# Decay and phase sums: matrix products replaced by scans with features on partitions, in a fused attention and MLP kernel

## The reference

```python
for t in range(S):
    new_re = ar * S_re - ai * S_im
    new_im = ar * S_im + ai * S_re
    kv = np.einsum('bhd,bhe->bhde', k[:, :, t], v[:, :, t])
    S_re, S_im = (new_re + kv, new_im)
    y[:, :, t] = np.einsum('bhd,bhde->bhe', q[:, :, t], S_re)
```

## Time and profile before

| what | value |
|---|---|
| three runs | 1012.15, 1011.91 and 1009.15 us, median 1011.91 |
| the profiled execution | 1009.13 us, its span 1007.3 us |
| mean granted TensorE clock | 0.989 |
| TensorE, matmul busy | 960.0 us, 95% of the span |
| VectorE, ScalarE, GpSimd busy | 528.4, 422.3 and 364.9 us |
| moved by DMA | 66.84 MB |

### The profile page before, as it was taken

The page is one execution under the profiler, slowest core; times in us unless marked ns, Lnnn a source line. Parts: engine busy times, 40 slices in busy tenths (PEclk is TensorE's granted clock), DMA queues, the critical chain, the costliest instruction groups (busy, mean ns, idle before and its releaser), DMA issues.

```text
span 1007.3 us, 15116 instructions
## 1 busy us (share of the span) xinstructions
PE 960.0 (95%) x5913; PEld 877.4 (87%) x5913; DVE 528.4 (52%) x669; ACT 422.3 (42%) x674; POOL 364.9 (36%) x296
## 2 busy tenths in 40 slices
PE   6887699999999999999999999999999999999997
PEld 3556699999999999999999999999888888888886
DVE  5669869669669669669669654242212121212110
ACT  4364554554555554554554533363222121212121
POOL 0353543543543552543553533253222222222221
PEclk9999799999999999999999999999999999999999
DMA  9254411311311221221221020421001010101000
GB/s 352 69 167 117 149 40 41 104 46 40 98 53 40 84 68 40 79 71 41 71 80 40 24 79 25 160 99 42 15 1 63 1 63 1 63 1 63 1 32 33
DMA packets 55913, 66.84 MB, mean 66 GB/s; under 512 B 4896, under 2 KB 50208, under 8 KB 55840
## 3 DMA queue, kind: packets, MB, share of 16 engines
q1 hardware_dynamic: 55840, 65.84, 20.5%
HBM read 45.37 MB, written 11.01 MB: 56 GB/s over the span
## 4 chain that ended last, share of the span: by engine, by line
PE 80%; issue 7%; DVE 5%; ACT 3%; POOL 3%; DMA 1%; SPq 1%; ACTq 0%; POOLq 0%; DVEq 0%
PE acc L737 15%; PE hb L717 14%; PE hb L916 10%; PE acc L938 8%; PE bR L916 5%; PE bQ L916 5%; PE bR L830 3%; POOL gL L1310 3%; PE bP L938 2%; PE bR L801 2%; PE acc L864 2%; PE bQ L801 2%; PE bQ L823 2%; PE bQ L820 2%; PE bQ L784 1%
## 5 line engine op out<-in xcount | busy, mean ns | idle before, releaser
L1310 POOL TENSOR_TENSOR gL<-g_sb,gH 128x384 fp32r<-128x384 f32 x128 | 155.4, 1214 | 253.5 <-ACT gH L1016 209.5
L717 PE MATMUL hb<-xHL,winH 128*128 128x384 f32 x768 | 162.8, 347 | 3.9 <-DMA xHL<-yHL 3.9
L1358 POOL TENSOR_TENSOR pL<-p_sb,pH 128x512 fp32r<-128x512 f32 x48 | 67.0, 1395 | 232.0 <-ACT pH L1098 232.0
L717 PEld LDWEIGHTS hb<-xHL,winH 128*128 128x128 f32 x768 | 133.6, 191 | 5.0 <-DMA xHL<-yHL 4.6
L1230 DVE SCALAR_TENSOR_TENSOR g_sb<-t_sb,hb 128x384 f32<-128x384 f32 x128 | 70.2, 549 | 123.7 <-ACT t_sb L1034 72.1
L737 PE MATMUL acc<-gH,woutH 128*128 128x384 f32 x384 | 129.1, 336 | 4.1 <-ACT gH L1016 2.6
L737 PE MATMUL acc<-gH,woutL 128*128 128x384 f32 x384 | 128.6, 335 | 0.0
L737 PE MATMUL acc<-gL,woutH 128*128 128x384 f32 x384 | 128.3, 334 | 0.0
L1034 ACT ACTIVATE t_sb<-hb,cst 128x384 f32<-128x384 f32 x128 | 74.5, 582 | 89.7 <-PE hb L717 89.5
L1016 ACT CAST gH<-g_sb 128x384 fp32r<-128x384 f32 x128 | 65.4, 511 | 86.5 <-DVE g_sb L1230 85.7
L717 PE MATMUL hb<-xHL,winL 128*128 128x384 f32 x384 | 87.7, 336 | 0.0
(11 more groups left out here) (163 smaller groups left out, 2000.2 us busy)
## 6 DMA issues: line engine op xcount, KB each, us to landing
xHL<-yHL SPq DMA_DIRECT2D x48, 144.0 KB, 2.6
AR<-in_a_re_dram SPq DMA_DIRECT2D x8, 576.0 KB, 3.9
AI<-in_a_im_dram SPq DMA_DIRECT2D x8, 576.0 KB, 5.1
q_sb<-in_q_dram SPq DMA_DIRECT2D x24, 192.0 KB, 2.5
...
```

The lines of the kernel that those rows point to most:

```text
L717: mm = pe.matmul(o, w[:, kk * DF1 + ft * P:kk * DF1 + (ft + 1) * P], xv(u)[:, 2 * kk + part, :], start=(i == 0), stop=(i == 8))
L1310: pool.tensor_tensor(gL[:, (n % 3) * UNIT:(n % 3 + 1) * UNIT], g_sb[:, :], gH[:, (n % 3) * UNIT:(n % 3 + 1) * UNIT].bitcast(F32), ALU.subt ...
L1358: pool.tensor_tensor(pL[:, (n % 3) * UNIT2:(n % 3 + 1) * UNIT2], p_sb[:, (n % 2) * UNIT2:(n % 2 + 1) * UNIT2], pH[:, (n % 3) * UNIT2:(n % ...
```

## The change

The preparation is laid out with **features on partitions** and tokens along the columns (inputs `a_re_x`, `a_im_x`, `qk_x` are laid out so outside the kernel). A sum over tokens is then a scan along the columns on VectorE: three of 384 columns for the decays and three for the angles of a unit, in `pre` steps 6 and 10. `decay_sums`, `halves_sums`, `angle_sums`, `TQ` and the transposes on VectorE are gone. q and k are decayed and turned in whole units of 1152 columns (GpSimd, steps 10, 11 and 13; VectorE, step 13). Per chunk, `scatter` issues ten SBUF to SBUF DMAs that sort the rows of QKc and QKs into a tile F with one head per column block; scores and output read F. k is still transposed (six 128-row transposes, `TK`), and `U` makes 16 products, the cosine part of k on one half of the columns and the sine part on the other. For the last chunk of a batch `TK` and `U` are left out. A chunk now has three stages (TK, S, YU), every 4 slots, in slots 1 to 11. Steps 1 to 13 of `pre` for unit u + 2 stand in slots 1 to 13. The staging buffers are gone: weight pieces land in the place of their low part; w_out pieces are requested when the w3 products are finished; GpSimd makes all eight low parts.

```diff
+        SPLIT_H = {(-2, 8): (0,), (-2, 9): (1,), (-2, 10): (2,), (-2, 13): (3,), (-1, 9): (4, 5), (-1, 10): (6, 7)}
+        SPLIT_L = {(-2, 14): (0,), (-1, 2): (1,), (-1, 5): (2,), (-1, 8): (3,), (-1, 10): (4,), (-1, 11): (5,), (-1, 12): (6,), (-1, 13): (7,)}
+        def steps(u, sl):
+            if u == -2:
+                return [(0, sl)]
+            if u == -1:
+                return [(1, sl + 1)] if sl < 9 else []
+            if u == 0:
+                return ([(1, sl + 10)] if sl < 4 else []) + ([(2, sl - 2)] if sl >= 3 else [])
+            return [(u + 2, sl)] if u + 2 < NU else []
...
+        W3_MM = {-2: {5: 40}, -1: {0: 3, 1: 3, 2: 3, 3: 3, 4: 2, 5: 2, 6: 2, 7: 2, 8: 4}}
+        W3_COPY = {(-2, 14): (0, 1), (-2, 15): (2, 3, 4), (-1, 3): (5,), (-1, 6): (6,), (-1, 8): (7,)}
...
+        STAGE = {"TK": 0, "S": 1, "YU": 2}
+            if not -1 <= u < NU - 1:
+                return None
+            first, step = {-1: (0, 3), 0: (4, 4)}.get(u, (1, 4))
+            j, r = divmod(sl - first - STAGE[stage], step)
+            return CPU * (u + 1) + j if r == 0 and 0 <= j < CPU else None
...
+            def scatter(g):
+                p, c = divmod(g, CPU)
+                sp.wait_ge(s["cos_rotated"], 2 * (p + 1))
+                sp.wait_ge(s["sin_rotated"], 2 * (p + 1))
+                if g >= 2:
+                    sp.wait_ge(s["y_summed"], g - 1)
+                else:
+                    sp.wait_ge(s["pads_cleared"], PADS)
+                landed = s[f"f_dma{g % 2}"]
+                f = qk(F[g % 2])
+                for src, r in ((QKc, 0), (QKs, YM)):
+                    b = cjn(src, QK)[:, :, c, :]
+                    sp.dma_start(f[r:r + D, 0:3, :], b[0:D, :, :]).then_inc(landed, 16)
+                    sp.dma_start(f[r:r + D, 3:6, :], b[D:D2, :, :]).then_inc(landed, 16)
+                    sp.dma_start(f[r:r + P - D2, 6:8, :], b[D2:P, 0:2, :]).then_inc(landed, 16)
+                    sp.dma_start(f[r + P - D2:r + D, 6, :], b[D2:D2 + 16, 2, :]).then_inc(landed, 16)
+                    sp.dma_start(f[r + P - D2:r + D, 7, :], b[D2 + 16:P, 2, :]).then_inc(landed, 16)
...
+                if i >= PIECES // 2:
+                    sp.wait_ge(s["w3_row_summed"], FT2)
...
+                    if u == -1 and sl == 8:
+                        for i in range(PIECES // 2, PIECES):
+                            load_w(i)
+                    if (g := chunk(u, sl, "YU")) is not None:
+                        if g % CPU == 0:
+                            scatter(g + 2)
+                        if g + 2 < NC:
+                            load_v(g + 2)
+                        if g % CPU == 0 and g + CPU < NC:
+                            load_q(g // CPU + 1)
+                    if (g := chunk(u, sl, "TK")) is not None and g % CPU == CPU - 1 and g + 1 < NC:
+                        load_k(g // CPU + 1)
+                    for p, t in steps(u, sl):
+                        if t == 12 and p + 1 < NU:
+                            load_a(p + 1)
+                        if t == 13:
+                            scatter(CPU * p)
+                            scatter(CPU * p + 1)
...
+            def TK(g):
+                if last_of_batch(g):
+                    return
+                p, c = divmod(g, CPU)
+                pe.wait_ge(s["scores_masked"], 2 * g)
+                pe.wait_ge(s["state_added"], carried(g))
+                for src, bk, sname in ((QKc, bQ, "cos_rotated"), (QKs, bR, "sin_rotated")):
+                    pe.wait_ge(s[sname], 2 * (p + 1))
+                    for j in range(KT):
+                        mm = pe.transpose(bk[:, j * P:(j + 1) * P], cjn(src, QK)[:, j, c, P:2 * P], IDENT)
+                    mm.then_inc(s["kT_psum"], 1)
+            def Sc(g):
+                pe.wait_ge(s[f"f_dma{g % 2}"], f_landed(g))
+                if last_of_batch(g):
+                    pe.wait_ge(s["scores_masked"], 2 * g)
+                    pe.wait_ge(s["state_added"], carried(g))
+                    if not last_of_batch(g):
+                        pe.wait_ge(s[("kc_copied", "ks_copied")[i]], 3 * (carried(g) + 1))
...
+                for b, h in enumerate(POS):
+                    for r, kk in enumerate((Kc, Ks)):
+                        mm = pe.matmul(bR[YM * r:YM * (r + 1), b * D:(b + 1) * D], kk[:, h * D:h * D + YM],
+                                       heads(v_sb[g % 2][:, :], h, D), start=True, stop=True)
...
+                if t == 7:
+                    act.wait_ge(s["log_r_centred"], p + 1)
+                    act.activation(mid_decay[:, :], blocks(W1)[:, :, P // 2 - 1], ACT.Exp).then_inc(s["mid_decays"], 1)
+                if t == 8:
+                    act.wait_ge(s["atan_num"], p + 1)
+                    act.activation(AI[:, :], AR[:, :], ACT.Exp).then_inc(s["q_decays"], 1)
+                    act.activation(AR[:, :], AR[:, :], ACT.Exp, scale=-1.0).then_inc(s["k_decays"], 1)
...
+                if t == 12:
+                    act.wait_ge(s["turns_wrapped"], p + 1)
+                    act.activation(W2[:, :], W1[:, :], ACT.Sin, scale=TWO_PI).then_inc(s["sin_turns"], 1)
+                    act.activation(W3[:, :], W1[:, :], ACT.Abs).then_inc(s["turns_abs"], 1)
+                    act.wait_ge(s["turns_abs"], p + 1)
+                    act.activation(W3[:, :], W3[:, :], ACT.Sin, scale=-TWO_PI, bias=HALF_PI).then_inc(s["cos_turns"], 1)
+                    act.preload_act_table_set("natural_log_exp_and_others")
...
-                    if n is not None and sl in EARLY_G:
+                    if n is not None:
+                        for p, t in steps(u, sl):
+                            pre(p, t)
                         high_g(n)
...
                 if t == 5:
...
+                    dve.wait_ge(s["log_r"], p + 1)
+                    dve.wait_ge(s["half_turn"], p + 1)
+                    dve.tensor_scalar(AR[:, :], W1[:, :], MIN_LOGR, None, ALU.max).then_inc(s["log_r_clipped"], 1)
+                    dve.tensor_reduce(least[:, p:p + 1], W1[:, :], AXIS.X, ALU.min).then_inc(s["least_log_r"], 1)
+                if t == 6:
...
+                    for j in range(KT):
+                        o = slice(j * UNIT, (j + 1) * UNIT)
+                        dve.tensor_tensor_scan(W1[:, o], keep[:, :], AR[:, o], 0.0, ALU.mult, ALU.add).then_inc(s["log_r_summed"], 1)
+                    dve.wait_ge(s["log_r_summed"], KT * (p + 1))
+                    dve.tensor_tensor(blocks(AR), blocks(W1), blocks(W1)[:, :, P // 2 - 1:P // 2].broadcast_to([P, KT * CPU, P]),
+                                      ALU.subtract).then_inc(s["log_r_centred"], 1)
...
+                    for j in range(KT):
+                        o = slice(j * UNIT, (j + 1) * UNIT)
+                        dve.tensor_tensor_scan(W1[:, o], ONE_C.broadcast_to([P, UNIT]), W2[:, o],
+                                               total[:, j:j + 1] if p % 2 else 0.0, ALU.mult, ALU.add).then_inc(s["turns_summed"], 1)
...
+                if t == 13:
+                    cos = blocks(W3)
+                    for i, sname in enumerate(("q_decayed", "k_decayed")):
+                        dve.wait_ge(s["cos_turns"], p + 1)
+                        dve.wait_ge(s[sname], p + 1)
+                        dve.tensor_tensor(qkv(QKc)[:, :, i, :], qkv(QKs)[:, :, i, :], cos, ALU.mult).then_inc(s["cos_rotated"], 1)
...
+                if t == 1 and p > 1:
+                    pool.wait_ge(s["a_dma"], 32 * (p + 1))
+                    pool.wait_ge(s["sin_rotated"], 2 * p)
+                    pool.tensor_tensor(W2[:, :], AI[:, :], AI[:, :], ALU.mult).then_inc(s["squares"], 1)
+                    pool.wait_ge(s["sin_turns"], p)
+                    pool.tensor_tensor(W1[:, :], AR[:, :], AR[:, :], ALU.mult).then_inc(s["squares"], 1)
+                for t_, i, gg, ready, landed, done in ((10, 0, AI, "q_decays", "q_dma", "q_decayed"),
+                                                       (11, 1, AR, "k_decays", "k_dma", "k_decayed")):
+                    if t == t_:
+                        pool.wait_ge(s[ready], p + 1)
+                        pool.wait_ge(s[landed], 16 * (p + 1))
+                        pool.tensor_tensor(qkv(QKs)[:, :, i, :], qkv(QKs)[:, :, i, :], blocks(gg), ALU.mult).then_inc(s[done], 1)
+                if t == 13 and p > 0:
+                    pool.wait_ge(s["sin_turns"], p + 1)
+                    for i in range(2):
+                        pool.wait_ge(s["cos_rotated"], 2 * p + 1 + i)
+                        pool.tensor_tensor(qkv(QKs)[:, :, i, :], qkv(QKs)[:, :, i, :], blocks(W2), ALU.mult).then_inc(s["sin_rotated"], 1)
...
-            EARLY_LOW = (0, 12, 13)
```

695 lines of the change are left out of this document (270 added, 425 removed).

## The result

The changed kernel takes **1076.24 us** (median of four runs, 1074.41 to 1079.04), the kernel before 1011.72 on the same chip. The ratio is **1.0646**, 95% interval 1.0612 to 1.068: 64.5 us slower, where 36 were forecast.

What follows compares the result with a forecast made beforehand. TensorE's streamed columns were taken to bound the units. Start +3, unit 0 +10, five units +27.5 (67.7 work plus 14 stalls against 76.2 each) and unit 6 -4.5 gave +36: 1048 us, 3.6% slower, range 985 to 1080.

Steps and rivals of the forecast that it cites:

- slot 5: Step 5 in each unit: copies of transposed k queue behind VectorE's preparation, holding the scores' second half; stall 1.8 us.
- slot 10: Step 10 in each unit: turns, scans and GpSimd's q product stand ahead of a mask TensorE needs; stall 4 us.
- slot 12: Step 12 in each unit: ScalarE's 6.1 us of sine work between relu and cast delays the low part; stall 2.4 us.
- slot 13: Step 13 in each unit: GpSimd's two products stand ahead of the low part of block 14; stall 3.7 us.
- TensorE's work in a unit: Units of three chunks: 8.5 us of 76.2 removed, leaving 67.7 us; k-v product left at 1.4 us.
- Clock: Lower clock after stalls above 2 us: some 1.2 us each, kept for the range, not in the sum.
- The start, +3: Ahead of unit 0: first hidden product at 113 us instead of 110.2, +3 us.
- Unit 0, +10: Unit 0: w_out low parts, 17 preparation steps and chunk 3's rotation and DMAs add 10 us to 80.8; without luck 17.
- In unit 7 ... the change touches nothing: Unit 7 and the second MLP behind it: no change in time.
- Clock and locks add up: Rival, chance 0.12: clock losses and slower scans add 3 us a unit, start and unit 0 at upper counts; about 1075 us.
- The scatter is late in the units too: Rival, chance 0.05: scores of each unit's first chunk wait 1 to 3 us for DMAs; 1055 to 1060 us.
- TensorE stays the bound: Rival, chance 0.25: stalls stay at 2 to 4 us a unit, below the work removed; about 970 us.

## Why the prediction was right, and where it was wrong

- **Direction and mechanism in the units: right.** The waits stand in the slots that the prediction followed, for what it said. By size: slots 2 and 3 0.5 forecast, 0.34 in every second unit; slot 5 1.8, 1.07 to 1.67; slot 6 2.0, 1.5; slot 10 4, 2.7 to 3.4; slot 12 2.4, 2.24; slot 13 3.7, 2.0 to 2.2 and once 3.56. In all 14, measured 10.5. The waits for the masks and the copies went when VectorE's order alone was changed, and the wait of slot 10 shrank by 2.2 us when the q product was left out, which shows the exclusion there. In slot 12 the first wait fell from 2.24 to 0.33 us without the cosine, as ScalarE's rows had it; what that is worth in time is half open.
- **TensorE's work in a unit: 67.7 forecast.** The 403.7 us of the five units, less 52.7 of waits and an estimated 21 at the lower clock (by the mean granted clocks 0.92, 0.94, 0.96, 0.94 and 0.98), leave 66.0 a unit. A part of the difference, some 0.9 us a unit, is the k-v product, which I had left at 1.4 us:

```profile
84.97 0.21 PE L854 MATMUL bR<-v_sb,Kc 128*64 128x48 f32 x1
...
85.99 0.59 PE L866 MATMUL acc<-wo_sb,w3t_sb 128*128 128x384 f32 x1
```

  1.02 us: the two column halves overlap, but not wholly (half of 1.39 would be 0.7).
- **Clock: kept for the range only, and wrong so.** An estimated 1.6 to 6.7 us a unit, 4.2 in the mean, went at the lower clock and belong in the sum. They made up for stalls and work that I had put too high: 67.7 + 14 = 81.7 was forecast, 66.0 + 10.5 + 4.2 = 80.7 is the mean. That the units' number came out is luck: terms were off with opposite sign.
- **The start, +3: wrong.** The step that failed is "the chain of step 1 to 13 ... scores 0 at 70". I counted the scatter's 6.1 us as a price for chunks 0 and 2, and did not ask what else stands behind it on SyncE's queue. The W3 rows did: 8.8 us. Two more things went the same way: the stores of x of chunk 2 stood behind the w_out requests (9.0 us at the first hidden product with the order turned round, though no time was won by it alone), and ScalarE's high part of the second output waited 6 us for the stores of the first one behind the scatter. The lock of VectorE behind GpSimd's low parts was forecast as +10; it measured 9.5 in its rows, 11 in the first hidden product.
- **Unit 0, +10: mis-sized**; 22.8, above even the count without luck (17). I named each piece (w_out low parts, 17 steps, rotation and ten DMAs of chunk 3) and took less than their sum. TensorE's waits in it sum to 25.6 us: among them 3.57 for hswish, 2.83 for the low part, 2.16 and 4.43 for the rotated k of chunk 3, 2.67 for F, 3.06 for the copies, 6.02 for a mask. Its mean granted clock is 0.88, where it was 0.96.
- **"In unit 7 ... the change touches nothing": wrong**, 6 us. The diff drops `EARLY_G` and with it the place of `high_g` behind the casts of w1, w2 and w3. The term stood in the printed diff and I read it for the units only.
- **The range.** 1076 us lies 4 us under the upper end of 985 to 1080. That end had been drawn for clock, scans and upper counts, and a good part of what filled it was unit 7 and a queue that I had not thought of: that the range held is in part luck.
- **The rivals.** "Clock and locks add up" named 1075 us, the time that came, but by +15 in the units; they gave less than the forecast. Its price for start and unit 0 (8 and 17) was nearer than mine. "The scatter is late in the units too" happened once in five units (3.6 us). That TensorE stays the bound needs another order of the steps, with one square moved to ScalarE: with them a unit takes 70.2 us.
